# Grouping the weight loads of a fused decayed-attention, MLP and mixture-of-experts kernel, and letting GpSimd take three decays of the first group in place of five

## The chip, the cores and the metric

The kernel runs on one core of a Trainium2 chip. The metric is the device time of one execution in microseconds. The kernel before takes 451.7 us (median of 3 runs, 450.69 to 452.8).

## What is computed

```python
def _attn_ref(r, k, v, w, u):                 # B, H, S, D = 2, 8, 768, 48
    state = np.zeros((B, H, D, D))
    for t in range(S):
        kt, vt, rt, wt = (k[:, :, t], v[:, :, t], r[:, :, t], w[:, :, t])
        cur = np.einsum('bhd,bhe->bhde', u[None] * kt, vt)
        y[:, :, t] = np.einsum('bhd,bhde->bhe', rt, state + cur)
        state = wt[:, :, :, None] * state + np.einsum('bhd,bhe->bhde', kt, vt)
...
    x = attn_out.transpose(0, 2, 1, 3).reshape(B * S, H * D)      # 1536 x 384
    x = np.maximum(x @ w_in, 0.0) ** 2 @ w_out                    # d_ff 2048
...
    expert_idx = np.argmax(x @ w_gate, axis=1)                    # 8 experts, capacity 384
    h = np.maximum(np.einsum('ecd,edf->ecf', disp, w1), 0.0)      # disp: each expert's rows, F 1024
    y = np.einsum('ecf,efd->ecd', h, w2)
    out[i] = gate_w[i] * y[expert_idx[i], pos[i]]
```

Everything is float32. Three stages follow each other: a recurrence over the sequence with a decay `w` (the attention), an MLP with a squared ReLU, and a layer of eight experts, each of which serves the rows whose largest gate logit is its own.

## The kernel before, in words

**Tiles.** The 1536 rows are cut into six groups of 256, and a group into two tiles `t` of 128 rows. For each tile the attention is computed in seven levels: a first level, five halvings (`level`, line 662, its matmuls on line 672) and transposed keys (`kk_rows`, matmuls on line 634), after which come products, increments of the state and outputs (lines 693, 705, 728). Between levels, keys and receptances are multiplied by the product of the decays of half a block: `update` on VectorE (line 1256, all heads of a tile, tile `KS`). In group 0 alone, GpSimd shares this work: `first_update` (line 566) does the last quarter of the columns for levels 1 to 5 and counts `upd_last`, VectorE the other three quarters and counts `upd`; TensorE waits for both before the level. `first_totals` (line 557) makes the products of decays of group 0 on GpSimd.

**MLP.** Sixteen slots of hidden columns per group: nine float32r matmuls for the hidden tile (line 753), ReLU, square and split in high and low half on ScalarE and VectorE, then six matmuls of the projection (line 767). From group 1 on, attention of the next group is woven in. All weights are loaded as float32 in chunks of 768 KB; ScalarE writes the high half (`W`, line 1019), VectorE the low half (line 1230) and counts `wl_ready`.

**Experts.** At run time each engine reads the number of rows of expert `e` and branches: up to 128 rows take `hidden_small` (line 948), more than that `hidden2` (eight tiles `f` of nine matmuls, line 933), and more than 256 both. `outputs2` (lines 980 and 987) follows once, twice or three times. On these inputs experts 1, 2, 3 and 5 take the small path, experts 4 and 6 two blocks, experts 0 and 7 three. The code of each path stands in the instruction stream, so that an expert of few rows jumps over the others' blocks. `hidden2` has three banks: tile `f` waits until the low half of tile `f - 3` (`hl_ready`) is taken. ScalarE does the ReLU of each tile (line 1165), and after the third tile (`f == 2`) the high half of the expert's own last weight chunk (`split_high_expert(e, CH - 1)`); VectorE takes the low halves (line 1542).

**Order of the loads.** SyncE issues all of them from one list. At the start: the two tiles of group 0, weight chunk 0 of the MLP, and then, each released by a step of group 0's updates, chunks 1 to 3, `v` and the tiles of group 1 (lines 398 to 413). For the experts, chunk `n` holds quarter `n % 4` of expert `n // 4`; 11 buffers (`RAW`) hold them in turn, so that chunk `n` waits until chunk `n - 11` is split (`wl_ready`). After expert `e` SyncE issues the gathered rows of expert `e + 2` (`load_rows`, line 477, each waits for `gt_ready`, which VectorE counts when it has taken the rows of expert `e + 1` over) and then four chunks (`load_part`, line 442):

```python
            for e in range(NE):
                n = CH * (e + 1) + RAW
                for m in range(MT):
                    load_rows(e + 2, m)
                for c in range(CH):
                    load_part(n + c)
```

Of the kernel before, what the change touches and what calls it, by code (L numbers as in the profile page):

```python
# [5 lines left out]
def rwkv_moe_kernel(nc, cap, dims, krw, v, u, w_in, w_out, w_gate, w1, w2, gate_rows, out):  # L6
# [8 lines left out]
    NE, _, FE = w1.shape  # L15
    HP = H // 2
# [4 lines left out]
    MT = cap // P  # L21
    CAP = MT * P
    C = 64
    NL = 6
# [4 lines left out]
    CH = 4  # L29
# [3 lines left out]
    RAW = CX + NRAW  # L33
# [16 lines left out]
    LAST_DOTS = (3, 3, 4, 4, 5, 5, 6, 6, 7, 7, 8, 8, 9, 9, 10, 10)  # L50
    PL = 3
    NCH = 4 + 3 + 1 + 2
    assert H * D == DM and cap % P == 0 and P == 2 * C and 1 << NL == C and DM == 3 * P and MT == 3
    assert 2 * SW == DM

# [3 lines left out]
    with ctx:  # L59
# [5 lines left out]
        def sem(name):  # L65
            return ctx.enter_context(nc.semaphore(name))
# [155 lines left out]
        upd = [sem(f"upd{n}") for n in range(2)]  # L222
        upd_last = [sem(f"upd_last{n}") for n in range(2)]
# [32 lines left out]
        xt2_done, xh2_ready, xl2_ready = sem("xt2_done"), sem("xh2_ready"), sem("xl2_ready")  # L256
# [9 lines left out]
        def need(eng, s, n):  # L266

            if not (isinstance(n, int) and n <= 0):
                eng.wait_ge(s, n)
# [113 lines left out]
        def _(sp):  # L383
            def load_tile(i, t):
                need(sp, xt_done[t], i - 1)
                need(sp, end_ready, 2 * (i - 2) + t + 1)
                for lo, hi, s in ((0, 2 * XW, ld_kr), (2 * XW, 3 * XW, ld_wd)):
                    sp.dma_start(KRW[t][i % 2][:, lo:hi], krw[2 * i + t, :, lo:hi]).then_inc(s[t][i % 2], 16)

            def load_v(i, t):  # L390
                need(sp, mid_read, 2 * (i - 2) + t + 1)
                sp.dma_start(VV[t][i % 2][:, :, :, :], v[2 * i + t]).then_inc(ld_v[t][i % 2], 16)


            def load_first(n):
                sp.dma_start(staged(n, mlp_chunk(n)[2]), mlp_chunk(n)[0]).then_inc(ld_w[n], 16)
# [1 line left out]
            load_tile(0, 0)  # L398
            load_tile(0, 1)
            load_first(0)  # L400
            sp.wait_ge(upd[1], 1)
            load_first(1)
            sp.wait_ge(upd[0], 2)
            for t in range(2):
                load_v(0, t)
            sp.wait_ge(upd[0], 3)
            load_first(2)
            sp.wait_ge(upd[0], 4)
            load_tile(1, 0)
            sp.wait_ge(upd[0], 5)  # L410
            load_first(3)
            sp.wait_ge(kn_ready[0], 1)
            load_tile(1, 1)
# [24 lines left out]
            def load_part(n):  # L438
                if n < CH * NE:
                    src, _, parts = expert_chunk(n // CH, n % CH)  # L440
                    sp.wait_ge(wl_ready, NW0 if n < RAW else NW0 + n - RAW + 1)
                    sp.dma_start(unsplit(n, parts), src).then_inc(ld_raw[n % RAW], 16)
# [41 lines left out]
                    load_part(RAW)  # L484
            for c in range(1, CH):
                load_part(RAW + c)
            for e in range(NE):
                n = CH * (e + 1) + RAW
                for m in range(MT):
                    load_rows(e + 2, m)  # L490
                for c in range(CH):
                    load_part(n + c)
            for m in range(MT):
                sp.wait_ge(scat2[m], 16 * NE)

# [2 lines left out]
        def _(pool):  # L498
# [61 lines left out]
            def first_update(t, l):  # L560

                pool.wait_ge(att[t], l + 1)
                pool.wait_ge(tot[t], l)
                need(pool, upd_last[t], l - 1)
                x, td = halves(0, t, l, HP - 1, HP), totals_of(0, t, l, HP - 1, HP)
                nc.gpsimd.tensor_tensor(x, x, td, ALU.mult).then_inc(upd_last[t], 1)

            for l in range(NL):
                for t in range(2):
                    first_totals(t, l)  # L570
                if l > 0:
                    for t in range(2):
                        first_update(t, l)

# [15 lines left out]
            def body(i, attn, mlp, gate):  # L590
                if gate:
# [8 lines left out]
                    for m in range(2):  # L600
                        pool.wait_ge(slot_ready, g + 1)
                        if g == NG - 1:
                            pool.wait_ge(gate_chain, NCH * NG)
                        pool.sem_inc(passed["pool"], 1)
# [26 lines left out]
        def _(pe):  # L631
# [5 lines left out]
            def right_of(x, c, l):  # L637

                return right_half(x[:, c:c + C], l)
# [18 lines left out]
            def level(i, t, l):  # L658
                pe.wait_ge(upd[t], NL * i + l)
                if i == 0:  # L660
                    need(pe, upd_last[t], l - 1)
                pe.wait_ge(sel[t], NMASK * i + l)
                if t == 0 and i >= 3 and l == NL - 1:
                    pe.wait_ge(rank_used, i - 2)
                x = KRW[t][i % 2]
                n = C - (1 << l)
                for q in range(HP):
                    for h in range(2):
                        for a in range(2):
                            rows, c = slice(DP * a, DP * a + D), q * P + h * C  # L670
                            to = half(h, a).start
                            last = nc.tensor.matmul(pair[t][to:to + n, a, q * P:q * P + C // 2],  # L672
                                                    x[rows, XW + c:XW + c + n], right_of(x[rows, 0:XW], c, l),
                                                    start=q == 0, stop=q == HP - 1)
                last.then_inc(att[t], 1)

            def kk_rows(i, t):
                pe.wait_ge(upd[t], NL * i + NL)
                if i == 0:
                    pe.wait_ge(upd_last[t], NL - 1)  # L680
                pe.wait_ge(sel[t], NMASK * (i + 1))
                pe.wait_ge(blk[t], i + 1)
                transposes(bank[2 * t + 1], KRW[t][i % 2][:, XW:2 * XW], HP, att[t])
# [541 lines left out]
        def _(dve):  # L1225
# [19 lines left out]
            def update(i, t, l):  # L1245
                if l == 0:
                    dve.wait_ge(ld_wd[t][i % 2], 16 * (i // 2 + 1))
                    dve.wait_ge(mixed_raw[t], i + 1)
                    dve.wait_ge(mixed_u[t], i + 1)
                else:  # L1250
                    dve.wait_ge(att[t], NSTEP * i + l + 1)
                    dve.wait_ge(upd[t], NL * i + l)
                    dve.wait_ge(tot[t], NL * i + l)
                q1 = HP - 1 if i == 0 and l > 0 else HP
                x = halves(i, t, l, 0, q1)
                tt(x, x, totals_of(i, t, l, 0, q1), ALU.mult).then_inc(upd[t], 1)  # L1256

# [99 lines left out]
            def choose(g):  # L1357
                n = [0]

                def link(ins):  # L1360
                    n[0] += 1
                    ins.then_inc(gate_chain, 1)
                    dve.wait_ge(gate_chain, NCH * g + n[0])

# [18 lines left out]
            def gate_value(g):  # L1383
                n = [4 if g < NG - 1 else NCH - 3]

                def link(ins):
                    n[0] += 1
                    ins.then_inc(gate_chain, 1)
                    dve.wait_ge(gate_chain, NCH * g + n[0])

# [6 lines left out]
                link(nc.vector.reciprocal(rows_of(g)[:, :, DM], den2))  # L1397
                assert n[0] == (7 if g < NG - 1 else NCH)

            def place(g):  # L1400
                n = [7 if g < NG - 1 else 4]

                def link(ins):
                    n[0] += 1
                    ins.then_inc(gate_chain, 1)
                    dve.wait_ge(gate_chain, NCH * g + n[0])

# [208 lines left out]
```

## Time and profile before

| | |
|---|---|
| median of 3 runs | 451.7 us (450.69 to 452.8) |
| the profiled execution | 451.77 us, span 450.0 us, mean granted TensorE clock 0.994 |
| TensorE matmul / weight load | busy 428.6 us (95%) / 406.7 us (90%) |
| VectorE, ScalarE, GpSimd | busy 303.2 us (67%), 257.7 us (57%), 63.4 us (14%) |
| DMA | 63.40 MB, mean 141 GB/s |
| experts | from 306.8 us to the end |

The span runs from the first to the last instruction; the device time of that execution is 1.8 us longer. In the rows below, a matmul group is one line of the kernel, "issue" is time in which an engine waited for nothing that the profile shows, and "[1.35 <-issue]" behind a row is idle time ahead of it and what ended it. SPq is SyncE's issuing of transfers.

### The profile page before, as it was taken

What the parts mean: (1) busy time and instruction counts of PE and PEld (TensorE: products, weight loads), DVE (VectorE), ACT (ScalarE), POOL (GpSimd) and SP (SyncE); (2) the same over time, 40 slices, a digit from 0 to 9 for tenths busy, and PEclk for the clock granted to TensorE, in tenths of its full rate; (3) what the DMA queues carried; (4) which work ended last, traced back from release to release, by engine and by line L of the source; (5) the groups of instructions that cost most, each with busy time, mean ns of one, the idle gap of its engine ahead of it and who ended that gap; (6) DMA issues with size and microseconds to landing.
All of it is one profiled execution on the core that took longest, in us unless ns stands there. A gap on an engine that the chain in (4) does not pass through costs nothing.

```text
span 450.0 us, 14551 instructions
## 1 busy us (share of the span) xinstructions
PE 428.6 (95%) x5882; PEld 406.7 (90%) x5882; DVE 303.2 (67%) x763; ACT 257.7 (57%) x527; POOL 63.4 (14%) x88
## 2 busy tenths in 40 slices
PE   3799999999999999999999999999999899999994
PEld 3678999999999999999999999989998789999994
DVE  6797866766777767777778638568548867687510
ACT  3366766546654664466446665573638766686421
POOL 8700000000000100010001000301031323421201
PEclk9999999999999999999999999999999989999999
DMA  7837886850400131010001093613785989520001
GB/s 240 300 102 244 309 296 243 308 225 3 167 31 1 39 133 65 3 37 2 4 1 39 2 358 136 204 60 94 284 297 165 353 280 300 172 62 2 30 2 45
DMA packets 35643, 63.40 MB, mean 141 GB/s; under 512 B 3980, under 2 KB 21950, under 8 KB 35568
## 3 DMA queue, kind: packets, MB, share of 16 engines
q1 hardware_dynamic: 33120, 57.87, 37.9%
q0 software_dynamic: 2304, 4.47, 2.7%
q8 instruction: 54, 0.88, 0.8%
q14 instruction: 21, 0.17, 0.1%
q10 hardware_dynamic: 144, 0.00, 0.0%
HBM read 50.77 MB, written 14.19 MB: 144 GB/s over the span
## 4 chain that ended last, share of the span: by engine, by line
PE 86%; POOL 3%; issue 3%; ACT 2%; DVE 2%; DMA 1%; POOLq 0%; SPq 0%; DVEq 0%; ACTq 0%
PE bank L767 22%; PE bank L753 22%; PE bank L980 6%; PE bank L933 5%; PE pair L672 5%; PE pair L634 4%; PE pair L948 3%; PE bank L948 3%; PE pair L933 3%; PE bank L987 3%; PE pair L693 2%; PE pair L728 1%; DMA stage<-in_moe_w_in 1%; PE pair L705 1%; PE pair L980 1%
## 5 line engine op out<-in xcount | busy, mean ns | idle before, releaser
L753 PE MATMUL bank<-XH,W 128*128 128x256 f32 x576 | 118.7, 284 | 0.1
L767 PE MATMUL bank<-W,GH 128*128 128x384 f32 x372 | 98.3, 345 | 0.2 <-issue 0.2
L753 PEld LDWEIGHTS bank<-XH,W 128*128 128x128 f32 x576 | 94.9, 189 | 1.1 <-issue 0.4
L753 PE MATMUL bank<-XL,W 128*128 128x256 f32 x288 | 80.6, 280 | 0.0
L1321 DVE TENSOR_TENSOR GL<-GG,GH 128x256 fp32r<-128x256 f32 x96 | 40.4, 421 | 35.1 <-ACT GH L1019 34.8
L1123 ACT ACTIVATE RB<-bank 128x256 f32<-128x256 f32 x96 | 36.6, 381 | 47.6 <-PE bank L753 47.1
L767 PEld LDWEIGHTS bank<-W,GH 128*128 128x128 f32 x372 | 61.7, 188 | 1.6 <-issue 0.4
L767 PE MATMUL bank<-W,GL 128*128 128x384 f32 x186 | 62.6, 336 | 0.0
L1019 ACT ACTIVATE GH<-GG 128x256 fp32r<-128x256 f32 x96 | 40.2, 418 | 34.1 <-PE bank L767 32.3
L753 PEld LDWEIGHTS bank<-XL,W 128*128 128x128 f32 x288 | 54.3, 189 | 0.0
L1256 DVE TENSOR_TENSOR KS<-KS 128x512 f32<-128x512 f32 (+1 forms) x72 | 48.9, 680 | 7.4 <-PE pair L672 7.2
L1230 DVE TENSOR_TENSOR W<-raw,W 128x1536 fp32r<-128x1536 f32 x23 | 40.1, 1753 | 9.5 <-ACT W L1019 9.5
L1283 DVE COPY_PREDICATED AD<-mask,pair 128x256 f32<-128x256 uint32 x48 | 24.4, 508 | 25.5 <-PE pair L672 25.4
L1129 ACT ACTIVATE GG<-RB 128x256 f32<-128x256 f32 x96 | 40.0, 416 | 2.1 <-DVE GL L1321 0.2
L980 PE MATMUL bank<-W,HH 128*128 128x384 f32 x192 | 39.0, 344 | 0.0
L672 PE MATMUL pair<-KS 48*62 48x32 f32 (+4 forms) x1920 | 33.8, 221 | 3.5 <-DVE KS L1256 1.7
L672 PEld LDWEIGHTS pair<-KS 48*62 48x62 f32 (+4 forms) x1920 | 29.9, 136 | 7.8 <-DVE KS L1256 2.4
L605 POOL DMA_INDIRECT slots<-X,slot_u x8 | 8.3, 1037 | 192.4 <-DVE slot_u L1427 178.3
L767 PEld LDWEIGHTS bank<-W,GL 128*128 128x128 f32 x186 | 34.9, 188 | 0.0
L620 POOL DMA_INDIRECT out<-x2T,GT x16 | 20.0, 1251 | 99.8 <-ACT x2T L1189 98.6
L1230 DVE TENSOR_TENSOR W<-stage,W 128x1536 fp32r<-128x1536 f32 x17 | 30.0, 1771 | 5.5 <-ACT W L1019 5.5
L1019 ACT ACTIVATE W<-raw 128x1536 fp32r<-128x1536 f32 x23 | 33.5, 1480 | 0.0
(165 smaller groups left out, 733.6 us busy)
## 6 DMA issues: line engine op xcount, KB each, us to landing
raw<-in_moe_w SPq DMA_DIRECT2D x23, 768.0 KB, 7.1
stage<-in_moe_w SPq DMA_DIRECT2D x9, 768.0 KB, 8.0
KS<-in_krw SPq DMA_DIRECT2D x12, 512.0 KB, 5.2
slots<-X SPq DMA_DIRECT2D x8, 579.0 KB, 7.8
VV<-in_v SPq DMA_DIRECT2D x12, 288.0 KB, 5.5
KS<-in_krw SPq DMA_DIRECT2D x12, 256.0 KB, 5.3
stage<-in_moe_w_in SPq DMA_DIRECT2D x4, 768.0 KB, 5.9
stage<-in_moe_w_out SPq DMA_DIRECT2D x4, 768.0 KB, 5.6
```

Of the source, the lines that this page charges most:

```text
L672: last = nc.tensor.matmul(pair[t][to:to + n, a, q * P:q * P + C // 2], x[rows, XW + c:XW + c + n], right_of(x[rows, 0:XW], c, l), start=q ...
L753: last = nc.tensor.matmul(bank[4 + f % 2][:, 0:2 * P], win[wa][:, c, f * P:(f + 1) * P], xa[:, c, :], start=n == 0, stop=n == 3 * KM - 1)
L767: last = nc.tensor.matmul(bank[6 + m][:, 0:DM], ga[(NF * g + f) % G3][:, cols], wout[wa][:, f, :], start=f == 0 and n == 0, stop=f == NF - ...
L933: last = nc.tensor.matmul(bank[HB[f % 3]][:, 0:2 * P], w1s(e, wa)[:, c, f * P:(f + 1) * P], xa[:, c, 0:2 * P], start=n == 0, stop=n == 3 * ...
L948: last = nc.tensor.matmul(bank[SMALL[m][c]][:, 0:CF], xa[:, k_, m * P:(m + 1) * P], w1s(e, wa)[:, k_, c * CF:(c + 1) * CF], start=n == 0, ...
L980: nc.tensor.matmul(y, HH[:, f, cols], w2s(e, wa)[:, f, :], start=f == 0 and wa == 0, stop=False)
L1019: return nc.scalar.activation(dst, src, ACT.Copy)
L1123: nc.scalar.activation(RB[:, :], bank[4 + f % 2][:, 0:2 * P], ACT.Relu).then_inc(relu_ready, 1)
L1129: nc.scalar.activation(GG[f % 2][:, :], RB[:, :], ACT.Square).then_inc(g_ready, 1)
L1230: return tt(parts[1], src, parts[0].bitcast(F32), ALU.subtract).then_inc(wl_ready, 1)
L1256: tt(x, x, totals_of(i, t, l, 0, q1), ALU.mult).then_inc(upd[t], 1)
L1321: tt(GL[k][:, :], GG[f % 2][:, :], GH[k][:, :].bitcast(F32), ALU.subtract).then_inc(gl_ready, 1)
```

## The change

It has three parts.

- **First attention, loads.** Chunk 1 of the MLP no longer waits for tile 1's first update (`upd[1] >= 1`) but for tile 0's second, together with `v`; chunk 2 waits for tile 0's fourth update in place of its third; tile 0 of group 1 and chunk 3 wait for the sixth, in place of the fourth and the fifth.
- **First attention, decays.** GpSimd shares levels 2, 3 and 4 (`SHARED`) in place of 1 to 5. VectorE does levels 1 and 5 in full width. GpSimd's share of level 2 waits for VectorE's update of level 1, and VectorE's level 5 for GpSimd's third share. TensorE loses some waits.
- **Experts, loads.** After the rows for expert `e + 2`, SyncE issues `AFTER[e]` chunks, 1, 2, 2, 4, 3, 5, 0, 0, in place of 4, 4, 4, 4, 1, 0, 0, 0. They also wait for `xt2_done`, the transposes of the rows of expert `e + 1`; `load_rows(e + 2, 2)` ahead of them already waits for something later.

```diff
+    SHARED = (2, 3, 4)
+    AFTER = (1, 2, 2, 4, 3, 5, 0, 0)
...
             load_first(0)
-            sp.wait_ge(upd[1], 1)
+            sp.wait_ge(upd[0], 2)
             load_first(1)
-            sp.wait_ge(upd[0], 2)
             for t in range(2):
                 load_v(0, t)
-            sp.wait_ge(upd[0], 3)
+            sp.wait_ge(upd[0], 4)
             load_first(2)
-            sp.wait_ge(upd[0], 4)
+            sp.wait_ge(upd[0], 6)
             load_tile(1, 0)
-            sp.wait_ge(upd[0], 5)
             load_first(3)
...
+            n = RAW + CH
             for e in range(NE):
-                n = CH * (e + 1) + RAW
                 for m in range(MT):
                     load_rows(e + 2, m)
-                for c in range(CH):
-                    load_part(n + c)
+                need(sp, xt2_done, MT * (e + 2) if AFTER[e] else 0)
+                for _ in range(AFTER[e]):
+                    load_part(n)
+                    n += 1
...
                 pool.wait_ge(att[t], l + 1)
                 pool.wait_ge(tot[t], l)
-                need(pool, upd_last[t], l - 1)
+                pool.wait_ge(upd[t], SHARED[0])
+                need(pool, upd_last[t], l - SHARED[0])
...
-                if l > 0:
+                if l in SHARED:
                     for t in range(2):
                         first_update(t, l)
...
                 if i == 0:
-                    need(pe, upd_last[t], l - 1)
+                    need(pe, upd_last[t], min(l - SHARED[0], len(SHARED)))
...
                 pe.wait_ge(upd[t], NL * i + NL)
-                if i == 0:
-                    pe.wait_ge(upd_last[t], NL - 1)
...
-                q1 = HP - 1 if i == 0 and l > 0 else HP
+                q1 = HP - 1 if i == 0 and l in SHARED else HP
+                if i == 0 and l == SHARED[-1] + 1:
+                    dve.wait_ge(upd_last[t], len(SHARED))
```

SyncE's list in the first attention, before (`stage` 0 to 3 are the MLP's chunks, `KS` the tiles of group 1, `VV` is `v`; what a row waits for stands behind it):

```order
L396 DMA stage1<-in_moe_w_out 128x4x384 [waits upd1]
L392 DMA VV00<-in_v 128x576 [waits upd0]
L392 DMA VV10<-in_v 128x576
L396 DMA stage2<-in_moe_w_in 128x3x512 [waits upd0]
L388 DMA KS0<-in_krw 128x1024 [waits upd0]
L388 DMA KS0<-in_krw 128x512
L396 DMA stage3<-in_moe_w_out 128x4x384 [waits upd0]
```

And with the change:

```order
L398 DMA stage1<-in_moe_w_out 128x4x384 [waits upd0]
L394 DMA VV00<-in_v 128x576
L394 DMA VV10<-in_v 128x576
L398 DMA stage2<-in_moe_w_in 128x3x512 [waits upd0]
L390 DMA KS0<-in_krw 128x1024 [waits upd0]
L390 DMA KS0<-in_krw 128x512
L398 DMA stage3<-in_moe_w_out 128x4x384
```

The order of the transfers is the same; four groups are left where there were five releases.

SyncE's list at the end of experts 3 to 5, before (`XG` and `X2` are the gathered rows, `raw` and `stage` the weight chunks). Chunk 27, the last quarter of expert 6, is the first `raw` row here:

```order
L477 DMA X2<-slots 128x386 [waits gt_ready2]
L442 DMA raw<-in_moe2_w2 128x4x384 [waits wl_ready]
L442 DMA raw<-in_moe2_w1 128x3x512 [waits wl_ready] x2
L442 DMA raw<-in_moe2_w2 128x4x384 [waits wl_ready]
L477 DMA XG0<-slots 128x386 [waits gt_ready0]
L477 DMA XG1<-slots 128x386 [waits gt_ready1]
L477 DMA X2<-slots 128x386 [waits gt_ready2]
L442 DMA raw<-in_moe2_w2 128x4x384 [waits wl_ready]
```

And with the change, at the end of expert 5, the last loads of the program:

```order
L477 DMA XG0<-slots 128x386 [waits gt_ready0]
L477 DMA XG1<-slots 128x386 [waits gt_ready1]
L477 DMA X2<-slots 128x386 [waits gt_ready2]
L442 DMA raw<-in_moe2_w2 128x4x384 [waits wl_ready,xt2_done]
L442 DMA raw<-in_moe2_w1 128x3x512 [waits wl_ready] x2
L442 DMA raw<-in_moe2_w2 128x4x384 [waits wl_ready] x2
```

Chunk 27 has moved from behind the rows of expert 5 to behind those of expert 7, and chunks 28 to 31 stand behind it.

GpSimd in the first attention, before (line 557 is `first_totals`, line 566 `first_update`):

```order
L557 TENSOR_TENSOR KS0<-KS0 128x128 [waits tot0]
L557 TENSOR_TENSOR KS1<-KS1 128x128 [waits tot1]
L566 TENSOR_TENSOR KS0<-KS0 128x2x32x2 [waits tot0,att0]
L566 TENSOR_TENSOR KS1<-KS1 128x2x32x2 [waits tot1,att1]
L557 TENSOR_TENSOR KS0<-KS0 128x64 [waits tot0]
L557 TENSOR_TENSOR KS1<-KS1 128x64 [waits tot1]
L566 TENSOR_TENSOR KS0<-KS0 128x2x16x4 [waits upd_last0,tot0,att0]
```

With the change:

```order
L560 TENSOR_TENSOR KS0<-KS0 128x128 [waits tot0]
L560 TENSOR_TENSOR KS1<-KS1 128x128 [waits tot1]
L560 TENSOR_TENSOR KS0<-KS0 128x64 [waits tot0]
L560 TENSOR_TENSOR KS1<-KS1 128x64 [waits tot1]
L570 TENSOR_TENSOR KS0<-KS0 128x2x16x4 [waits upd0,tot0,att0]
```

The two multiplies of level 1 are gone here, and so are the two of level 5 further down.

## Rows read from the trace of the kernel before

**Rows 1.** The page, busy time and share of the span.
```profile
PE 428.6 (95%) x5882; PEld 406.7 (90%) x5882; DVE 303.2 (67%) x763; ACT 257.7 (57%) x527; POOL 63.4 (14%) x88
```

**Rows 2.** Timeline of TensorE, first attention: start, us, what, count, [idle before <-releaser].
```profile
17.46 0.64 PE L672 MATMUL pair<-KS 48*32 48x32 f32 x26 [0.21 <-DVE KS L1256]
19.44 0.78 PE L672 MATMUL pair<-KS 48*32 48x32 f32 x38 [1.35 <-issue]
20.75 1.94 PE L634 MATMUL pair<-ident,KS 128*128 128x128 f32 x8 [0.52 <-POOL KS L566]
...
24.36 0.51 PE L705 MATMUL pair<-VV,KS 64*64 64x48 f32 x14
25.28 0.33 PE L705 MATMUL pair<-VV,KS 64*64 64x48 f32 x9 [0.41 <-issue]
```

**Rows 3.** The page, DMA queues: packets, MB, share of 16 engines' span.
```profile
q8 instruction: 54, 0.88, 0.8%
```

**Rows 4.** Timeline of SyncE's issues, first attention.
```profile
15.55 0.80 SPq L388 DMA_DIRECT2D KS<-in_krw  x2
17.43 0.38 SPq L396 DMA_DIRECT2D stage<-in_moe_w_out  x1
```

**Rows 5.** Who waited for whom, TensorE, experts: us in total, times, longest.
```profile
PE pair L948 <- DVE XL L1518: 0.8, 1, 0.8
PE bank L933 <- DVE XL L1518: 0.6, 1, 0.6
```

**Rows 6.** Chain of waits, experts: start, us, what.
```profile
356.08 1.61 issue
357.69 2.99 PE pair L948 x9
...
364.10 0.33 PE pair L634 x3
...
388.99 2.08 PE pair L948 x9
```

**Rows 7.** Windows: us, busy by engine (x), PEclk, DMA share, GB/s.
```profile
354.00:356.00 2.00, 1.89 (x11) 1.56 (x9) 2.00 (x5) 2.00 (x3) 0.00 (x0) 1.00 1.07 373
359.50:363.00 3.50, 3.50 (x10) 2.72 (x10) 1.64 (x1) 0.60 (x1) 2.89 (x3) 0.57 1.03 340
395.00:397.00 2.00, 2.00 (x13) 1.97 (x12) 1.32 (x5) 2.00 (x4) 0.00 (x0) 1.00 0.04 8
```

**Rows 8.** Instructions of line 1256 up to 25 us: ns min/median/max, starts, forms.
```profile
L1256 DVE TENSOR_TENSOR KS<-KS x12: 544/554/761, 5.6 to 20.3; 128x384 f32<-128x384 f32 x10, 128x512 f32<-128x512 f32 x2
```

**Rows 9.** Timeline of GpSimd at the first shared update.
```profile
11.01 1.19 POOL L566 TENSOR_TENSOR KS<-KS 128x128 f32<-128x128 f32 x2
```

**Rows 10.** Timeline of TensorE at the second halving.
```profile
11.57 1.83 PE L672 MATMUL pair<-KS 48*60 48x32 f32 x64 [0.94 <-DVE KS L1256]
```

**Rows 11.** Timeline of ScalarE, first attention, chunk 3 of the MLP.
```profile
26.66 1.48 ACT L1019 ACTIVATE W<-stage 128x1536 fp32r<-128x1536 f32 x1
```

**Rows 12.** DMA issues in short windows from 17.4, 385.3, 326.1: KB, us to landing.
```profile
stage<-in_moe_w_out SPq DMA_DIRECT2D x1, 768.0 KB, 6.7
...
raw<-in_moe_w SPq DMA_DIRECT2D x1, 768.0 KB, 5.0
...
raw<-in_moe_w SPq DMA_DIRECT2D x1, 768.0 KB, 6.3
```

**Rows 13.** Timeline of SyncE, end of expert 5.
```profile
399.81 0.32 SPq L477 DMA_DIRECT2D X<-slots  x1
```

**Rows 14.** Timeline of ScalarE, expert 6: last split, fourth ReLU.
```profile
403.06 1.48 ACT L1019 ACTIVATE W<-raw 128x1536 fp32r<-128x1536 f32 x1
404.43 0.38 ACT L1165 ACTIVATE HH<-bank 128x256 fp32r<-128x256 f32 x1
```

**Rows 15.** Timeline of VectorE, expert 6, the fourth low half.
```profile
405.20 0.42 DVE L1542 SCALAR_TENSOR_TENSOR HL<-bank,HH 128x256 fp32r<-128x256 f32 x1
```

**Rows 16.** Chain of waits, expert 6, sixth and seventh tile.
```profile
404.90 2.16 PE bank L933 x18
```

More of the change, by code:

```diff
@@ L486, in _ @@
                 load_part(RAW + c)
+            n = RAW + CH
             for e in range(NE):
-                n = CH * (e + 1) + RAW
                 for m in range(MT):
                     load_rows(e + 2, m)
-                for c in range(CH):
-                    load_part(n + c)
+                need(sp, xt2_done, MT * (e + 2) if AFTER[e] else 0)
+                for _ in range(AFTER[e]):
+                    load_part(n)
+                    n += 1
+            assert n == CH * NE
             for m in range(MT):
```

## The prediction

> **What bounds the kernel now.** I read the busy shares first: TensorE is busy for 428.6 of 450.0 us [rows 1]. So time is won or lost only where TensorE is idle or slow, and next I listed those places. The list of waits names next to nothing between the first attention, where group 0 has no MLP beside it, and the experts.
>
> In the first attention the timeline shows TensorE stopping for 1.35 us in the middle of a group of like matmuls, after 26 of 64, and for 0.41 us after 14 of the 64 of line 705 [rows 2]. "Issue" means that nothing was waited for: no data was missing. Between these points lie 38 + 8 + 64 + 14 = 124 matmuls with as many weight loads, 248 instructions and some waits. The queues hold one for instructions: 54 packets, 0.88 MB, so 16.3 KB each [rows 3], and TensorE runs 2 x 5882 matmuls and weight loads in all [rows 1], some 218 for a packet. I read both stops as the edge of a packet of instructions that came late. And it came late among data: SyncE had issued three transfers within 2 us ahead of the longer stop [rows 4].
>
> In the experts the waits name three stops, all where an expert with up to 128 rows ends and the code jumps on: 0.8 us ahead of expert 2, 0.6 us ahead of expert 4 [rows 5], and in the chain 1.61 us of issue ahead of expert 3 [rows 6]. TensorE's own idle time there is 1.8 us: it is busy for 1.89 of the 2.00 us up to 356 and starts again at 357.69 [rows 6, 7]. The same jump from expert 5 to 6 is on no list of stops. The windows tell why these may differ: the DMA engines' share was 1.07 ahead of expert 3, and 0.04 ahead of expert 6 [rows 7]. Behind the longest stop the granted clock drops: 0.57 on average from 359.5 to 363, so most of it at the lower of the two levels, 1.2 GHz; the two groups of nine of expert 3 take 2.99 us each where expert 5 needs 2.08 [rows 6, 7]. That is 1.8 us more.
>
> **The change, part by part.** The sum is made against the profiled execution, 451.77 us (span 450.0 and 1.8 around it), which is as good as the median, 451.7.
>
> *Loads of the first attention.* Today the packet that the group at 17.46 needs competes with chunk 2, both parts of a tile, issued at the fourth update (15.55), and chunk 3, at the fifth (17.43) [rows 4]. With the change, chunk 2 goes out at the fourth update and nothing more until the sixth, which is another 1.9 us behind the fifth, at about 19.3; by the fourth, chunk 1 and `v` have mostly passed. I take the stop of 1.35 as gone but for 0.05 and that of 0.41 as gone: -1.3 and -0.4. Bounds: both stay (0), both go (-1.76). What is late next is chunk 3, issued behind the tile, at about 19.7 on the new time. Its landing took 6.7 us [rows 12], so 26.4; its reader starts at 26.66 [rows 11], or 24.8 once everything is 1.9 earlier, and ends 1.6 later than it could. TensorE has nine filler matmuls of line 741 and the second tile's outputs in that time, so I charge 0.1; if nothing covers it, up to 0.7.
>
> The Trainium skill, "Runtime: NRT & Kernel Launch", section "Instruction fetch mechanics", says that engines fetch code in blocks of 256 instructions while they run the block before, and that a crossing is mostly hidden. By that rule these two stops would not be there to be removed and the two terms would be 0. The trace agrees with the size of the block (248 and the waits), and differs on the hiding: 1.35 us stood open.
>
> *Decays.* GpSimd loses four multiplies of 0.6 us each at first (1.19 for two [rows 9]). VectorE's four updates become 512 wide in place of 384: median 554 ns, longest 761 [rows 8], so at most 0.2 each. On the path: TensorE's second halving begins at 11.57 [rows 10], when GpSimd's first multiply (11.01 and half of 1.19) ends; it will begin when VectorE's wider update ends, some 0.4 earlier. At level 5, the transposes now wait for GpSimd (0.52 [rows 2]) and then for VectorE, 0.15 wider: as good as even. The delay at levels 2 to 4 stays. I take -0.3; bounds -0.7 (the whole of both waits is won) and +0.4 (two widenings in full on the path, nothing won).
>
> *Loads of the experts.* After expert 1, two chunks go out in place of four, and after expert 2 two, so in expert 2 the engines are free of data from about 351 on; the rows alone are left. The stops ahead of experts 2, 3 and 4 should go the way of the one ahead of expert 6, 0.8 + 1.8 + 0.6 = 3.2 [rows 5, 6]. VectorE's work on the next rows ends close to TensorE's there, so I leave 0.2: -3.0; bounds -3.2 and 0. With the long stop the lower clock goes: -1.8 (twice 2.99 less twice 2.08); bounds -1.8 and 0. The new wait for `xt2_done` costs nothing: the row loads ahead of it wait for VectorE's copy of the same rows. What stands behind it in SyncE's list is only weights. Of the other chunks 28 is the tightest, second in the last burst, and its reader stands at the end of expert 6.
>
> *Chunk 27 is the exception.* It is now issued behind the last row load at 399.81 + 0.32 [rows 13], about 400.2, with expert 6 already running. ScalarE wants it at 403.06, ahead of its fourth ReLU [rows 14]. Loads of this size landed 5.0 us after their issue where one went alone, 6.3 with others behind it [rows 12]; here four are behind it. So it lands at 405.2 to 406.5, and ScalarE is held for 2.1 to 3.4 us. The fourth ReLU (0.38) and the fourth low half (0.42 [rows 15]) follow, to about 405.3 plus that delay; the seventh tile waits for them and would start in the middle of the piece at 404.90, at 405.98 [rows 16]. TensorE idles 1.4 to 2.7 us. I take the upper part, +2.5, as the burst is long; both ends stay in the range. An idle time of 1.8 us brought the clock down in expert 3; 2.5 us should do so here: +1.7, between 0 and 1.8.
>
> **Sum:** first attention -1.3 - 0.4 + 0.1 - 0.3 = -1.9; experts -3.0 - 1.8 + 2.5 + 1.7 = -0.6; together -2.5, so 451.8 - 2.5 = **449.3 us**.
>
> **The rivals.** A measurement of this kernel can tell about 0.5% (2.3 us) from no change, so faster is below 449.4, slower above 454.0.
>
> *The clock holds in expert 6.* Then 1.7 is not paid: 447.6. For it: the two short stops, 0.6 and 0.8, did not lower it. Against: 1.8 did.
>
> *Chunk 27 is hidden.* With a landing under 3.6 us, neither the wait nor the clock costs anything: 449.3 - 4.2 = 445.1. Against: the fastest of the loads here took 5.0 [rows 12].
>
> *Half of it.* The late code packets go in one place and not in the other, since whatever moves the loads also moves the fetches: 451.8 - 0.6 = 451.2 with the first attention left as it is, 451.8 - 1.9 - 2.4 + 4.2 = 451.7 with the gain at the experts' jumps cut by half.
>
> *The jumps cost what they cost.* This is the one on the other side. The place is the end of experts 1 to 3: a jump past unused blocks needs code that nobody fetched ahead, however idle the DMA engines are. Then -3.0 and -1.8 fall away, while chunk 27 is late all the same: 451.8 - 1.9 + 4.2 = 454.1, and 456.0 if the first attention gains nothing. It decides from the point where less than 0.2 of the 3.2 us is won. For it: all three stops are at jumps. Against: the jump behind expert 5 is free at a DMA share of 0.04 [rows 7].
>
> The same section of the Trainium skill states this rule: a taken branch to code outside the window of two blocks forces a fetch that the engine waits for. The trace agrees at three jumps and disagrees at the fourth.
>
> **How the numbers follow.** The forecast has 0.40, the clock that holds 0.25, the hidden chunk 0.10, half of it 0.15, the jumps 0.10. Of the forecast I put 0.24 below 449.4, since it stands close to that line; with the next two nearly whole that makes 0.59 faster. "Half" and the rest of the forecast make 0.34 for the same; the jumps leave 0.07 for slower. The range of 8 in 10 reaches from 446.0, past the second case and half way to the third, to 452.5, past the half cases.
>
> **What the profile would show.** Right: no idle of over 0.5 us inside the groups of lines 672 and 705 before 25 us; the experts' stops under 0.3 us where they were 0.8, 1.8 and 0.6, and 2.1 us for each group of nine in expert 3; then ScalarE's split of chunk 27 waiting for a DMA for 2 to 3.4 us, and a stop of TensorE of 1.4 to 2.7 us ahead of the seventh tile of expert 6. Wrong: a stop at one of the three jumps with the DMA engines idle, a chunk 3 that ScalarE waits for beyond 1 us, or new stops at other packet edges, as in the bursts behind expert 3 and 5.

## The result, and the profile after

The changed kernel takes **457.4 us** (median of 4 runs, 456.45 to 458.98), the kernel before 451.6 in the same sitting: ratio 1.013, interval 1.0093 to 1.0167. Slower, where the forecast was 449.3 us and faster. The profiled execution took 458.98 us, span 457.2, mean granted clock 0.981; it is the longest of the four, so that the profiles of before and after differ by 7.2 us where the medians differ by 5.8. Executions more than 1.5% above the fastest of their kernel are left out of the ratios: two of the ten of x3 below. Lines after the change stand a few higher: 672 is 676, 705 is 707, 634 is 638, 933 is 935, 948 is 950, 980 is 982, 1019 is 1021, 1256 is 1260, 1542 is 1546, 654 (group 1's first level) is 658.

The page's busy shares of the kernel after:

```profile
PE 433.6 (95%) x5882; PEld 411.0 (90%) x5882; DVE 303.9 (66%) x763; ACT 257.4 (56%) x527; POOL 59.1 (13%) x84
```

The same instructions on TensorE as before [rows 1], 5.0 us more of busy time: part of the loss is the clock and not idle time. GpSimd has four instructions less.

Who waited for whom, TensorE, kernel after (us in total, times, longest):

```profile
PE bank L935 <- DVE HL L1546: 2.8, 1, 2.8
...
PE pair L707 <- issue: 2.0, 1, 2.0
...
PE pair L950 <- issue: 1.9, 1, 1.9
...
PE pair L676 <- issue: 1.1, 1, 1.1
```

No wait at lines 933 and 948 for VectorE's rows is left [rows 5]; the stops named "issue" are not gone, and one for a low half is new.

Timeline of TensorE, first attention, kernel after (start, us, what, count, [idle before <-releaser]):

```profile
17.15 0.64 PE L676 MATMUL pair<-KS 48*32 48x32 f32 x26 [0.16 <-DVE KS L1260]
18.89 0.78 PE L676 MATMUL pair<-KS 48*32 48x32 f32 x38 [1.10 <-issue]
...
26.09 0.92 PE L707 MATMUL pair<-VV,KS 64*64 64x48 f32 x49 [2.02 <-issue]
...
35.06 0.69 PE L658 MATMUL pair<-KS 48*64 48x64 f32 x32 [0.25 <-ACT KS L1021]
```

The same place before, the last of these rows:

```profile
31.70 0.69 PE L654 MATMUL pair<-KS 48*64 48x64 f32 x32 [0.27 <-ACT KS L1019]
```

The stop of 1.35 us is now 1.10, that of 0.41 is now 2.02 [rows 2]. By 17.15 the new kernel was 0.31 ahead (TensorE's second halving starts at 10.94, 0.63 earlier than in [rows 10]; half of that is kept); at 26.09 it is 0.81 behind; at group 1's first level it is 3.36 behind. The other 2.55 are work at the lower clock: TensorE has no wait over 0.25 us in between. Windows of the kernel after (us, busy by engine, PEclk, DMA share, GB/s):

```profile
24.00:26.00 2.00, 0.07 (x6) 0.00 (x0) 1.76 (x1) 0.12 (x1) 0.00 (x0) 1.00 0.98 330
...
30.00:32.00 2.00, 2.00 (x29) 1.56 (x31) 0.90 (x2) 0.00 (x0) 0.00 (x0) 0.50 0.00 0
```

TensorE stood still with the DMA engines full, and then ran at 1.2 GHz (PEclk 0.50) to about 33.75, where before it ran at 2.4. What SyncE had issued by then, kernel after:

```profile
15.18 0.38 SPq L398 DMA_DIRECT2D stage<-in_moe_w_in  x1
19.99 0.80 SPq L390 DMA_DIRECT2D KS<-in_krw  x2
20.83 0.43 SPq L398 DMA_DIRECT2D stage<-in_moe_w_out  x1
21.92 0.81 SPq L390 DMA_DIRECT2D KS<-in_krw  x2
```

The last two issues are the second tile of group 1, which the kernel before sends at 22.49. That group of loads has left its place ahead of the first stop [rows 4] and stands ahead of the second. Chunk 3 reached its reader at 27.74 in place of 26.66 [rows 11], with 0.18 us of wait for it.

The first matmul of expert 0 (line 933, now 935) starts at 309.59 in place of 305.60 (not 306.8, as the table of the profile before has it): 3.99 behind, of which 3.36 are from the first attention and 0.63 from the MLP in between; where in it they arise stays open. From one expert's first matmul to the next one's (TensorE's timeline):

| from, to | before | after |
|---|---|---|
| 1, 2 | 11.48 | 10.50 |
| 2, 3 | 12.62 | 12.79 |
| 3, 4 | 13.02 | 12.23 |
| 4, 5 | 18.12 | 18.05 |
| 5, 6 | 10.50 | 10.69 |
| 6, 7 | 18.05 | 22.76 |

Expert 0 (28.03) and expert 7 (32.6) are as before. The sum is +3.2, and +7.2 with the start: the whole difference of the spans. Chain of waits, kernel after, expert 3 and expert 6 (start, us, what):

```profile
359.29 1.62 issue
360.91 3.73 PE pair L950 x9
...
403.38 5.72 DMA raw<-in_moe_w
...
409.13 1.48 ACT W L1021
...
411.40 1.34 PE bank L935 x9
```

The jump to expert 3 costs what it did: TensorE idles for 1.95 us, of which 1.62 stand in the chain, and the lower clock follows (3.73 for nine matmuls, in place of 2.99 [rows 6]). In expert 6 stands chunk 27. Its issue and its burst, SyncE and the DMA issues of the window 403 to 405, kernel after:

```profile
403.38 3.20 SPq L442 DMA_DIRECT2D raw<-in_moe_w  x5
```
```profile
raw<-in_moe_w SPq DMA_DIRECT2D x4, 768.0 KB, 10.5
```

The five chunks go out at 403.38 to 405.75; the median of 10.5 is over those that have a landing on record, the third and the fourth. Chunk 27, the first, took 5.72 by the chain. It went out 1.50 us behind the first matmul of expert 6 (401.88), where the forecast had 0.87. ScalarE and VectorE, kernel after:

```profile
409.13 1.48 ACT L1021 ACTIVATE W<-raw 128x1536 fp32r<-128x1536 f32 x1 [3.36 <-DMA raw<-in_moe_w]
```
```profile
410.92 0.42 DVE L1546 SCALAR_TENSOR_TENSOR HL<-bank,HH 128x256 fp32r<-128x256 f32 x1 [3.03 <-ACT HH L1167]
```

From the split ScalarE goes on to the fourth ReLU, as in [rows 14], and TensorE waits 2.8 us for its low half. The clock is at 1.2 GHz behind it:

```profile
412.60:416.00 3.40, 3.40 (x18) 3.40 (x17) 1.97 (x5) 1.43 (x4) 0.00 (x0) 0.50 1.06 370
```

### The profile page after: what moved, and what is told of

Same layout as the page of the kernel before. It is cut to its first block, busy times and chain, and to the rows that moved or that the text cites. A ratio compares the mean times of both kernels' runs of the same rounds, so it can differ in the third digit from the quotient of the medians.

```text
span 457.2 us, 14553 instructions
## 1 busy us (share of the span) xinstructions
PE 433.6 (95%) x5882; PEld 411.0 (90%) x5882; DVE 303.9 (66%) x763; ACT 257.4 (56%) x527; POOL 59.1 (13%) x84
## 4 chain that ended last, share of the span: by engine, by line
PE 86%; DMA 4%; issue 3%; DVE 3%; ACT 3%; SPq 1%; POOLq 0%; DVEq 0%; ACTq 0%
PE bank L769 22%; PE bank L755 21%; PE bank L982 6%; PE pair L676 5%; PE bank L935 4%; PE pair L638 4%; PE pair L950 3%; PE bank L989 3%; PE bank L950 3%; PE pair L935 3%; PE pair L730 2%; PE pair L695 2%; DMA stage<-in_moe_w_in 1%; PE pair L707 1%; ACT W L1021 1%
## 5 line engine op out<-in xcount | busy, mean ns | idle before, releaser
L1325 DVE TENSOR_TENSOR GL<-GG,GH 128x256 fp32r<-128x256 f32 x96 | 40.3, 420 | 33.2 <-ACT GH L1021 32.8
```

Of the source, the lines that this page charges most:

```text
L1325: tt(GL[k][:, :], GG[f % 2][:, :], GH[k][:, :].bitcast(F32), ALU.subtract).then_inc(gl_ready, 1)
```

## The experiments

Each kernel was timed beside the kernel before on the same chip. Ratios are to that kernel, with their 95% interval; they can differ by up to 0.3% from the quotient of the medians. The kernel before itself went from 449.9 to 456.9 us in these executions, and each kernel has one profile (the whole change two), so a stop's length in one profile can't be taken for the kernel's.

**x1, x2: the first attention's two parts alone.** x1 is the kernel before with the new order of the first loads:

```diff
-            sp.wait_ge(upd[1], 1)
+            sp.wait_ge(upd[0], 2)
             load_first(1)
-            sp.wait_ge(upd[0], 2)
...
-            sp.wait_ge(upd[0], 3)
+            sp.wait_ge(upd[0], 4)
             load_first(2)
-            sp.wait_ge(upd[0], 4)
+            sp.wait_ge(upd[0], 6)
             load_tile(1, 0)
-            sp.wait_ge(upd[0], 5)
             load_first(3)
```

> The kernel before with the new order of the loads in the first attention alone. Theory (a packet of TensorE's code is fetched half a packet ahead and queues behind the data in flight): the stop in the group of line 705 grows from 0.41 to about 2.0 us, since the tile of group 1 and chunk 3 now move when that packet is asked for, and the clock falls behind it; time +3 to +4 us. Rival (it is GpSimd's new share that costs the time): within 1 us of before.

x2 has the three decays (`SHARED`, with the waits that belong to them) and nothing else of the change:

```diff
-                if l > 0:
+                if l in SHARED:
```

> The kernel before with GpSimd sharing levels 2 to 4 alone. Theory (packets and data): within 1 us of before, both stops stay at about 1.3 and 0.4 us. Rival (the share costs the time): +3 us.

Measured: x1 452.64 us, 1.0019 (0.9991 to 1.0047); x2 452.31, 1.0001 (0.9978 to 1.0023). Timeline of TensorE, x1:

```profile
18.73 0.78 PE L670 MATMUL pair<-KS 48*32 48x32 f32 x38 [0.62 <-issue]
...
25.11 0.96 PE L703 MATMUL pair<-VV,KS 64*64 64x48 f32 x50 [0.82 <-issue]
```

and x2:

```profile
24.84 0.92 PE L705 MATMUL pair<-VV,KS 64*64 64x48 f32 x49 [1.20 <-issue]
```

Neither theory held in its stops: x1 was to have 2.0 us at the second and +3 to +4 us, and x2 was to keep 1.3 and 0.4, where its first stop is gone. The clock holds in both. The new loads alone don't cost what they cost in the whole change. How little one profile says is shown by three more with the first attention of the kernel before: x3 and x9 have 1.62 and 1.36 at the first stop, 0.42 and none at the second, but x6 has 0.61 and 1.10. So the stops of x1 and x2 stand within what happens without a change.

**x10: the two together**, with the experts' loads of before (both edits above).

> The changed kernel with the experts' loads as before: the first attention's loads and GpSimd's share together. Apart they gave 1.002 and 1.000 of the time before. Theory (they meet: with both, the last group of loads is in flight just when the packet for line 705 is asked for, the stop there comes to about 2 us and the clock falls behind it): +2 to +3.5 us on before. Rival (they add): within 1 us of before.

Measured: 455.88 us, 1.0097 (1.0066 to 1.0127). Timeline of TensorE, x10:

```profile
19.23 0.78 PE L672 MATMUL pair<-KS 48*32 48x32 f32 x38 [0.69 <-issue]
...
26.43 0.92 PE L703 MATMUL pair<-VV,KS 64*64 64x48 f32 x49 [1.66 <-issue]
...
34.34 0.69 PE L654 MATMUL pair<-KS 48*64 48x64 f32 x32 [0.25 <-ACT KS L1017]
```

1.002 and 1.000 alone, 1.010 together. The second stop is 1.66, and the granted clock fell behind it (0.61 and 0.54 in the windows 28 to 30 and 30 to 32, where x1 has 1.00). This isn't one profile's chance: the four profiles with both parts (x10, x4 and two of the whole change) have 1.66 to 2.02 there, all others at most 1.20. Group 1's first level starts at 34.34 to 35.63 us in these four, at 31.24 to 32.11 in the kernel before, x1, x2, x3 and x9, and at 33.54 in x6. In x10 the whole difference of the spans (3.3 us) is there before the experts begin (3.65 at the first matmul of expert 0); its stop of 2.1 us ahead of expert 3 is the one of 1.8 in the kernel before.

**Why a stop grows.** The instruction queue (q8) can be seen packet by packet. Windows of 1 us of the DMA view; kernel before from 17, x9 (below) from 399:

```profile
q8 instruction: 1, 0.02, 5.9%
```
```profile
q8 instruction: 1, 0.02, 7.1%
```

One packet in each. Starts read from the trace in this way stand so to TensorE's going on ("again" is the second profile of the whole change):

| kernel, stop | packet starts | TensorE goes on | difference | stop |
|---|---|---|---|---|
| before, first | 17.16 | 19.44 | 2.28 | 1.35 |
| after, first | 16.46 | 18.89 | 2.43 | 1.10 |
| x1, first | 16.32 | 18.73 | 2.41 | 0.62 |
| x2, first | 14.97 | | | none here |
| x5, first | 15.07 | | | none |
| x12, first | 14.72 | | | none |
| x6, first | 16.59 | 18.86 | 2.27 | 0.61 |
| before, second | 22.98 | 25.28 | 2.30 | 0.41 |
| x1, second | 22.68 | 25.11 | 2.43 | 0.82 |
| x2, second | 22.36 | 24.84 | 2.48 | 1.20 |
| x6, second | 23.05 | 25.51 | 2.46 | 1.10 |
| x9, second | 22.32 | | | none |
| x10, second | 24.12 | 26.43 | 2.31 | 1.66 |
| again, second | 24.17 | 26.75 | 2.58 | 1.94 |
| after, second | 23.77 | 26.09 | 2.32 | 2.02 |

TensorE goes on 2.2 to 2.6 us after its packet starts, whatever the kernel; this holds for all the "issue" stops over 0.3 us inside pieces of code in the thirteen profiles. The stop is decided by when the packet starts and when TensorE gets to the edge, and a stop is absent where the packet starts early. With one tile in two parts and a chunk issued at 20.0 to 20.8 and the second tile at 21.9, the packet of the second stop started at 23.77. But x1 issued the same loads 0.1 to 0.3 us earlier, and its packet started at 22.68. No row says when a packet is asked for, so why both parts together make it start at 23.5 to 24.2 is not shown; half a packet ahead, as the theories have it, is an assumption.

**x5: first loads one by one**, in the kernel before.

```diff
-            sp.wait_ge(upd[0], 3)
-            load_first(2)
             sp.wait_ge(upd[0], 4)
-            load_tile(1, 0)
+            load_first(2)
             sp.wait_ge(upd[0], 5)
-            load_first(3)
+            load_tile(1, 0)
             sp.wait_ge(kn_ready[0], 1)
+            load_first(3)
```

> The kernel before with other gaps in the first attention: chunk 2 at the fourth update, the tile of group 1 at the fifth, chunk 3 with the second tile of group 1 behind the transposed keys. Theory: the packet asked for at about 16.1 us moves at once, the stop in the group of line 672 falls from 1.35 to about 0.5 us (2.3 us from the packet's start to TensorE's going on, less 1.8 us for half a packet of matmuls), the one of line 705 stays near 0.4; -0.8 us. Price: chunk 3 may hold ScalarE up to 1 us. Rival (stops of this kind do not hang on data): stop of 1.35 stays.

Measured: 451.21 us, 0.9974 (0.9945 to 1.0003), which is not clear of no change. Neither stop is there, but chunk 3 is late: ScalarE waits 2.70 us for it, and TensorE for ScalarE:

```profile
PE pair L633 <- ACT KS L1018: 2.0, 1, 2.0
```

**x3: the experts' loads alone.**

```diff
+    AFTER = (1, 2, 2, 4, 3, 5, 0, 0)
...
-                for c in range(CH):
-                    load_part(n + c)
+                for _ in range(AFTER[e]):
+                    load_part(n)
+                    n += 1
```

> The kernel before with the new order of the experts' loads alone. Theory: +3 us, as -0.8 and -0.6 at the jumps to experts 2 and 4, 0 at the jump to expert 3, and +4 to +5 in expert 6, where chunk 27 is waited for and the clock falls. Rival (the jumps cost what they cost): stops of 0.8, 1.8 and 0.6 all stay, time +4.5 us.

Measured: 454.76 us, 1.0054 (1.0023 to 1.0086). Who waited for whom, x3:

```profile
ACT W L1022 <- DMA raw<-in_moe_w: 4.1, 1, 4.1
...
PE bank L936 <- DVE HL L1545: 3.5, 1, 3.5
```

and its chain:

```profile
344.89 2.08 PE pair L951 x9
...
355.68 2.31 PE pair L951 x9
```

Here all three jumps are free, the one to expert 3 against the theory (10.51, 10.95 and 10.68 us from experts 1, 2 and 3 to the next, where before had 11.48, 12.62 and 13.02), a gain of 5.0 us; expert 6 takes 24.33 in place of 18.05, 6.3 more, of which the wait is 3.5 and the clock most of the rest (at half from 403.8 to 410.7).

**x4: chunk 27 one burst earlier**, in the changed kernel.

```diff
-    AFTER = (1, 2, 2, 4, 3, 5, 0, 0)
+    AFTER = (1, 2, 2, 4, 4, 4, 0, 0)
```

> The changed kernel with chunk 27 issued after expert 4 in place of expert 5, four chunks after each. Theory: expert 6 has neither a stop ahead of its seventh tile nor a fall of the clock; 4.5 to 5 us faster than the changed kernel, so +1 us on the kernel before; the price could be a stop at the jump to expert 6, up to 1 us, as one more chunk is in flight in expert 5. Rival (the stop in expert 6 is a late packet of code and not chunk 27): the stop stays, time as changed, +5.8 us.

Measured: 452.74 us, 1.0021 (0.9991 to 1.005). Expert 6 is back at 18.11, no wait for a low half. The price is there too: 0.47 us at the jump to expert 6, and 11.13 us from expert 5 to 6 in place of 10.50. One chunk moved by one burst is worth some 1% of the kernel. The stop of 1.9 at the second edge of the first attention and the one at the jump to expert 3 (1.7) are still there.

**The change once more**, beside these.

> The changed kernel itself, once more beside the others. Every theory: 1.010 to 1.016 of before; expert 6 waits for chunk 27 and the clock falls. Open is whether the stop at the jump to expert 3 (1.95 us in the first profile, none in the kernel with the experts' loads alone) is there in each execution.

Measured: 457.29 us, 1.0116 (1.0066 to 1.0166). The same places again, with other sizes; behind the stop at the jump to expert 3 the clock held this time:

```profile
PE bank L935 <- DVE HL L1546: 3.4, 1, 3.4
PE pair L707 <- issue: 2.1, 2, 1.9
PE pair L950 <- issue: 1.7, 1, 1.7
```

**x9: data put in flight at the jump that was free**, in the kernel before. As x3, with

```diff
+    AFTER = (4, 4, 4, 0, 5, 0, 0, 0)
```

> The kernel before, with its weight chunks behind the experts' rows spread as 4, 4, 4, 0, 5 in place of four each: nothing goes out behind expert 3, and five chunks behind expert 4's rows, so that data are in flight at the jump from expert 5 to 6, which is free in the kernel before. Theory (a jump costs what the data queued in front of its instructions cost): a new stop of TensorE of 0.5 to 1.8 us appears at that jump, with or without the lower clock behind it; the jumps to experts 2 to 4 stay as they are, apart from the one to expert 5 or 4 that has lost its burst and is free. Time 0 to 3 us above before. Rival (the jump from 5 to 6 is free for a reason of its own, for instance its place in the code): no stop there, whatever is in flight.

Measured: 454.94 us, 1.0057 (1.0023 to 1.0091). Windows and TensorE's timeline, x9:

```profile
396.00:398.00 2.00, 2.00 (x14) 2.00 (x14) 1.72 (x4) 1.99 (x3) 0.00 (x0) 1.00 1.06 399
398.00:400.00 2.00, 2.00 (x14) 1.97 (x13) 1.60 (x1) 1.90 (x4) 0.00 (x0) 1.00 1.08 370
```
```profile
400.06 0.86 PE L990 MATMUL bank<-W,HL 128*128 128x384 f32 x4
402.94 0.36 PE L936 MATMUL bank<-XH,W 128*128 128x256 f32 x1 [2.02 <-DVE W L1233]
```

The stop is there, 2.02 us, with the lower clock behind it; from expert 5 to 6 it is 12.66 us in place of 10.50, from 6 to 7 19.60 in place of 18.05. The releaser named is a split on VectorE (401.15 to 402.90), so a late weight would explain it too. The kernel before speaks against that. TensorE, then VectorE:

```profile
398.63 0.86 PE L987 MATMUL bank<-W,HL 128*128 128x384 f32 x4
399.33 0.29 PE L933 MATMUL bank<-XH,W 128*128 128x256 f32 x1
```
```profile
399.70 1.75 DVE L1230 TENSOR_TENSOR W<-raw,W 128x1536 fp32r<-128x1536 f32 x1
```

There TensorE begins expert 6 ahead of that very split; the order on both engines is the same in x9, so expert 6 doesn't need it. Nor is the split itself late in x9: it stands 1.45 us behind the kernel before's (401.15 and 399.70), and so do the outputs of expert 5 (396.15 and 394.70). What differs is the instruction packet: in x9 it starts at 399.28, 3.1 us after the outputs of expert 5 began (396.15), in the kernel before at 395.0, 0.3 after (394.70). TensorE goes on 3.65 us after the packet's start; at the stops ahead of expert 3 this is 3.3 to 3.5 in nine profiles. The jump has no property of its own that makes it free.

**x6, x7, x12: the bursts put where they hurt least.** x6 is the kernel before with

```diff
+    AFTER = (3, 1, 2, 7, 0, 4, 0, 0)
```

so that chunk 27 goes out behind expert 3, and experts 1 and 2 are followed by few. x7 is x5 and x6 together. x12 is x6 with, in the first attention, chunk 2 and 3 as before and the tile behind them:

```diff
-            sp.wait_ge(upd[0], 4)
-            load_tile(1, 0)
             sp.wait_ge(upd[0], 5)
             load_first(3)
             sp.wait_ge(kn_ready[0], 1)
+            load_tile(1, 0)
             load_tile(1, 1)
```

> The kernel before with 3, 1, 2, 7, 0, 4, 0, 0 chunks after the experts: little in flight when experts 1 to 3 enter their output stage, chunk 27 in the burst behind expert 3. Theory: no stop at the jumps to experts 2, 3 and 4, nothing waited for in expert 6, clock high to the end; 4 to 5 us faster than before (ratio 0.990). Rival (the jumps cost what they cost): stops of 0.8, 1.8, 0.6 stay, time as before.

> The kernel before with both spacings that did something alone: the first attention's loads one by one (0.9974 of before alone) and the experts' chunks as 3, 1, 2, 7, 0, 4 (0.9925 alone). If the two places don't touch each other, the ratios multiply: 0.990, or 447 to 448 us. Rival: as with the two parts of the change in the first attention, they don't add; then it stays at 0.993 or above.

> The same experts' spacing (3, 1, 2, 7, 0, 4), and in the first attention chunk 3 goes out at the fifth update, ahead of both parts of the next tile, which wait for the first keys' norms. Theory: one transfer in front of the instructions that are asked for at about 16 us in place of three, so the stop of 1.35 us shrinks to 0.5 or less, and chunk 3 is no longer late (its reader waited 2.7 us in the version that sent it last); the next tile may be late by up to 1 us for group 1's first level. 446.5 to 448.5 us, ratio 0.987 to 0.992. Rival: the tile, issued last, is late by more than 2 us, and TensorE stops in line 658's level instead: 449 us or above.

Measured: x6 449.63 us, 0.9925 (0.9885 to 0.9966); x7 447.74, 0.9887 (0.9841 to 0.9932); x12 447.91, 0.9903 (0.9864 to 0.9941). In x6 the jumps take 10.45, 10.78 and 11.43, 4.5 us less than before, and expert 6 takes 18.06; 1.8 us of that are lost again in the first attention, whose code and loads are the kernel before's. In x7 chunk 3 is late as in x5 (TensorE waits 1.6 us for ScalarE, ScalarE 2.3 for the chunk); in x12 it isn't. x12's waits of TensorE:

```profile
PE pair L656 <- DVE XL L1318: 1.2, 1, 1.2
...
PE bank L769 <- issue: 1.1, 1, 1.1
```

Its granted clock never falls between 24 us and the last stretch. x6, x7 and x12 are faster than both kernels; their intervals overlap, so what the first attention's spacing adds is not shown.

## Why the prediction was wrong

**What bounds the kernel** was read rightly: TensorE is lost only where it stands or is slow, the stops named "issue" end 2.2 to 3.7 us after an instruction packet starts, by the place, and data in flight delay that start. x9 shows the last point as a cause at a jump, and with it the rival "the jumps cost what they cost" falls: all three are free in x3, and a free one could be made dear. The time it forecast, 454.1 to 456.0, lay nearest to the result for other reasons.

**First attention, -1.3 and -0.4: wrong, and the step that failed.** I had written "nothing more until the sixth" update and "I take the stop of 1.35 as gone but for 0.05 and that of 0.41 as gone". The bounds ran from 0 to -1.76 and held no loss. Measured: 1.10 and 2.02, +1.36 us, and the clock behind the second, +2.55 us. x10 has these edits without the experts' and lies 1.0% above the kernel before, so here is most of the miss. Three things were wrong. The loads that leave one packet edge have to go somewhere, and the next edge stands 124 matmuls on: I worked out that very distance and never laid the new issue times, which I had as well (19.3 and 19.7), beside it. Nor did spacing free the first edge: a packet that starts at 16.3 is still too late for it (x1). And the sum took loads and decays as independent, where neither costs anything alone (x1, x2) and both together do; how they meet stays open. "New stops at other packet edges" stood among the signs that would prove me wrong, with no price and no chance of its own.

The Trainium skill, "Runtime: NRT & Kernel Launch", section "Instruction fetch mechanics", has blocks fetched while the one before runs, a crossing being mostly hidden. The trace agrees in part: of the fifteen crossings in the table above, four are free, and at the eleven others 0.41 to 2.02 us stood open.

**Chunk 3, +0.1**: its reader came 1.08 later, with 0.18 of wait. TensorE was 0.8 us behind at 26.09 and fell further back, so the term costs nothing that can be seen.

**Decays, -0.3**: not shown. The profile has 0.31 at 17.15 us and x4 has 0.44, but in x2, x10 and the change once more the same group starts 0.30 to 0.45 later than in the kernel before. Line 1260 is wider as foreseen, with its median up to 25 us at 682 ns in place of 554 [rows 8]:

```profile
L1260 DVE TENSOR_TENSOR KS<-KS x12: 548/682/896, 5.7 to 19.9; 128x512 f32<-128x512 f32 x6, 128x384 f32<-128x384 f32 x6
```

Alone it made no difference in time (x2).

**Experts, -3.0 and -1.8**: too much. Expert 2's and 4's stops went, -0.98 and -0.79. The one of 1.8 ahead of expert 3 stayed with its clock. I had written that "the engines are free of data from about 351 on", which is 5.9 us behind expert 2's first matmul (345.07) and would be 354.1 in the kernel after. There they were still busy when its last outputs began, at 356.62:

```profile
352.00:354.00 2.00, 2.00 (x15) 1.53 (x14) 1.69 (x2) 1.10 (x2) 1.70 (x2) 1.00 1.00 331
354.00:356.00 2.00, 2.00 (x13) 2.00 (x14) 1.78 (x4) 1.92 (x3) 1.39 (x2) 1.00 0.84 289
356.00:358.00 2.00, 2.00 (x15) 1.96 (x14) 1.49 (x2) 1.95 (x4) 0.00 (x0) 1.00 0.65 188
```

x3 did win the -4.8 that I forecast (5.0). The same stretches of x3, as far behind the first matmul of expert 2:

```profile
348.61:350.61 2.00, 2.00 (x15) 1.54 (x14) 1.69 (x2) 1.10 (x2) 1.70 (x2) 1.00 1.02 386
350.61:352.61 2.00, 2.00 (x13) 2.00 (x14) 1.78 (x4) 1.92 (x3) 1.38 (x2) 1.00 1.03 388
352.61:354.61 2.00, 2.00 (x15) 1.96 (x14) 1.48 (x2) 1.94 (x4) 0.00 (x0) 1.00 0.44 107
```

The new wait for `xt2_done`, which I costed at nothing, is not to blame. In the kernel after the two chunks go out 0.88 and 1.31 us behind expert 2's first matmul, in x3, without that wait, at 1.42 and 1.90. What differs is how fast the same loads pass: 386 and 388 GB/s in x3, 331 and 289 in the kernel after. Where both have a landing on record, the second of the two chunks lands 8.5 us behind that matmul in x3, and 9.8 in the change once more and 10.4 in x4, which both have the stop. The packet starts at 7.6 in x3, and 9.0 to 9.4 with the stop. x3 has one profile, and why the loads are slower in the three others stays open; the forecast, which left the stop no more than 0.2, had no room for it.

**Chunk 27, +2.5, and the clock, +1.7**: right in mechanism and place. The wait of TensorE was 2.8 (3.4 and 3.5 in the other profiles), 0.1 to 0.8 above my 1.4 to 2.7, and the lower clock came: +4.7 in all, for +4.2 (+5.2 in the change once more, +6.3 in x3). Chunk 27 took 5.7 us to land, and 6.9 in the change once more, for 5.0 to 6.3. "The fastest of the loads here" wasn't 5.0: one of this size, issued at 376.75 in the kernel before, took 4.6.

In the sum, by the two profiles: -1.9 was +3.4, -4.8 was -1.5 (-3.4 in the change once more, where the clock held behind the jump), +4.2 was +4.7, and 0.6 in the MLP was not foreseen.

## What to carry to other kernels

Instruction packets start late when weights are in flight (x9). Before moving a load, mark in the trace where the packets of the bounding engine start (the DMA view in windows of 1 us) and lay the new issue times beside them, at the next edges as well as at the one that is to be freed. When a group of transfers is put off, find the one with the nearest reader and send it first or in the burst before; here one chunk was worth 1%. And parts of a change that touch the same stretch are measured together, for 1.002 and 1.000 made 1.010. Take a second profile before a stop's length is put down to an edit: with the same code and loads ahead of it, a stop was 1.35, 1.62, 1.36 and 0.61 us.

## What was not expected

TensorE goes on 2.2 to 2.6 us after its packet of 16 KB starts, and 3.3 to 3.7 at the jumps ahead of experts 3 and 6, though the packet itself took about 1 us. With three of its five chunks yet to land, a packet at a jump started 3.1 us after the last piece of code began (x9), in place of 0.3.

The granted clock fell behind stops of 1.9 us and more wherever it was high before (1.90 and 2.02 in x9, 2.02 and 1.95 in the kernel after, 2.1 in x10, 2.0 in x5), and between 1.5 and 1.8 it went both ways: it fell behind 1.80 (the kernel before), 1.66 (x10) and 1.55 (x7), and held behind 1.65 to 1.73 at the jump to expert 3 in x1, x4, x5 and the change once more. It stayed low for 3.4 us in most places, and for 6.8 in the first attention of the kernel after and in expert 6 of x3. It can also come late: in x4 and in the change once more it reached 2.4 GHz first at 32.1 and 33.2 us, in x6, with a stop of 1.1 us, at 29.9, where the kernel before, x1 and x2 have it from some 24 us. So a stop in the first attention costs more than its own length.
